# Two gated layers in split float32: every product as 64-row units in the two row tiles of TensorE

## What is computed

```python
x = causal_conv(x, softmax(weight, axis=-1))     # 4 x 4096 tokens of 192 features, 8 heads, 7 taps
h = x @ w_in1                                    # [16384, 192] @ [192, 2048]
x = (h * np.cos(h)) @ w_out1                     # [16384, 2048] @ [2048, 192]
h = x @ w_in2
out = (h * np.clip(h + 3.0, 0.0, 6.0) / 6.0) @ w_out2
```

## Time and profile before

| what | value |
|---|---|
| time, median of 3 runs | 2410.09 us (2410.08 to 2410.48) |
| the profiled execution's own time | 2408.54 us |
| its span, first to last instruction | 2406.8 us |
| mean granted clock of TensorE | 0.995 |
| matmuls | 10254 |
| weight loads | 10254 |
| DVE, ACT, POOL busy | 1776.7, 1495.7, 1313.7 us |
| moved by DMA | 32.8 MB, mean 14 GB/s |

### The profile page before, as it was taken

The page is one execution under the profiler, slowest core; times in us unless marked ns, Lnnn a source line. Parts: engine busy times, 40 slices in busy tenths (PEclk is TensorE's granted clock), DMA queues, the critical chain, the costliest instruction groups (busy, mean ns, idle before and its releaser), DMA issues.

```text
span 2406.8 us, 32826 instructions
## 1 busy us (share of the span) xinstructions
PE 2367.1 (98%) x10254; PEld 1929.2 (80%) x10254; DVE 1776.7 (74%) x2253; ACT 1495.7 (62%) x1748; POOL 1313.7 (55%) x543
## 2 busy tenths in 40 slices
PE   5999999999999999999999999999999999999998
PEld 3788888888888888888888888888888888888886
DVE  8777776777767777767777677777677776777753
ACT  4765566665666655666656666566666566665663
POOL 6755555555555555555555555555555555555554
PEclk8999999999999999999999999999999999999999
DMA  4100000000000000000000000000000000000001
GB/s 110 38 1 13 7 7 13 13 13 13 0 13 13 13 13 7 7 13 13 13 13 0 13 13 13 13 6 7 13 13 13 13 0 13 13 13 13 3 4 20
DMA packets 208226, 32.76 MB, mean 14 GB/s; under 512 B 203088, under 2 KB 207184, under 8 KB 208208
## 3 DMA queue, kind: packets, MB, share of 16 engines
q1 hardware_dynamic: 208208, 32.53, 7.7%
HBM read 19.92 MB, written 12.58 MB: 14 GB/s over the span
## 4 chain that ended last, share of the span: by engine, by line
PE 97%; DVE 1%; issue 1%; DMA 1%; SPq 0%; ACT 0%; POOL 0%; DVEq 0%; POOLq 0%; ACTq 0%
PE h_ps L347 10%; PE h_ps L346 10%; PE acc L366 10%; PE acc_tail L368 10%; PE h_ps L349 10%; PE acc L365 10%; PE acc_tail L369 10%; PE h_ps L348 10%; PE h_ps L350 10%; PE acc L367 10%; DMA gate<-in_moe_w_out 1%; DVE pre L520 0%; DVE gate L533 0%; DVE in_ftail L580 0%; DVE in_f L580 0%
## 5 line engine op out<-in xcount | busy, mean ns | idle before, releaser
L690 POOL TENSOR_TENSOR g_lo<-gate,g_hi 128x1024 fp32r<-128x1024 f32 x512 | 1270.2, 2481 | 1070.0 <-ACT g_hi L442 1069.7
L428 ACT ACTIVATE pre<-h_ps,three 128x1024 f32<-128x1024 f32 x256 | 286.7, 1120 | 547.0 <-PE h_ps L350 547.0
L442 ACT ACTIVATE g_hi<-gate 128x1024 fp32r<-128x1024 f32 x512 | 538.8, 1052 | 31.7 <-DVE gate L533 31.2
L520 DVE TENSOR_TENSOR pre<-pre,h_ps 128x1024 f32<-128x1024 int32 x256 | 311.9, 1218 | 257.3 <-ACT pre L426 257.3
L535 DVE SCALAR_TENSOR_TENSOR gate<-pre,h_ps 128x512 f32<-128x512 f32 x512 | 327.3, 678 | 214.5 <-ACT pre L428 213.5
L533 DVE TENSOR_TENSOR gate<-pre,h_ps 128x512 f32<-128x512 f32 x512 | 331.6, 685 | 129.4 <-ACT pre L436 126.0
L346 PE MATMUL h_ps<-in_hi,win_hi 128*128 128x512 f32 x1024 | 406.1, 397 | 18.7 <-DVE gate L533 9.9
L426 ACT ACTIVATE pre<-h_ps 128x1024 int32<-128x1024 f32 x256 | 262.4, 1025 | 232.5 <-PE h_ps L350 232.5
L347 PE MATMUL h_ps<-in_lo,win_hi 128*128 128x512 f32 x1024 | 406.1, 397 | 0.0
L349 PE MATMUL h_ps<-in_tail,wtail_hi 128*128 128x512 f32 x1024 | 403.4, 394 | 0.0
L366 PE MATMUL acc<-g_lo,wout 128*128 128x512 f32 x1024 | 402.6, 393 | 0.0
(11 more groups left out here) (69 smaller groups left out, 2225.8 us busy)
## 6 DMA issues: line engine op xcount, KB each, us to landing
x_in<-in_x SPq DMA_DIRECT2D x128, 64.0 KB, 2.2
out_dram<-o_blk SPq DMA_DIRECT2D x128, 64.0 KB, 1.8
blk_tail<-in_x SPq DMA_DIRECT2D x64, 64.0 KB, 2.2
out_dram<-blk_tail SPq DMA_DIRECT2D x64, 64.0 KB, 1.8
stage<-in_moe_w_out SPq DMA_DIRECT2D x6, 384.0 KB, 3.2
stage<-in_moe_w_in SPq DMA_DIRECT2D x3, 512.0 KB, 3.7
stage<-in_moe_w_in SPq DMA_DIRECT2D x6, 256.0 KB, 4.1
gate<-in_moe_w_out SPq DMA_DIRECT2D x2, 384.0 KB, 12.2
```

What stands on the lines that cost most here:

```text
L442: act.activation(g_hi[:, q % G_BUFS, :], gate[:, q % 2, :], ACT.Copy).then_inc(ghi_ready, 1)
L690: pool.tensor_tensor(g_lo[:, n, :], gate[:, q % 2, :], g_hi[:, n, :].bitcast(F32), ALU.subtract).then_inc(glo_ready, 1)
```

## The change

A matmul of 128 rows becomes two *units* of 64 rows: the lower ones use rows 64 to 127 (`LOW`), the upper ones rows 0 to 63 (`UP`), each with its own weight load. A slot has 19 *turns*; in each, a lower unit is issued and then an upper one, into different banks:

| turns | lower rows | upper rows |
|---|---|---|
| 0 to 2 | first product, half 0 (5 units, turns 0 to 4) | the last 3 tail units of the second product before |
| 3 to 8 | first product, half 1 (4 units, turns 5 to 8) | main second product, 6 units |
| 9 to 12 | tail of the second product, 4 units | first product, half 0, 4 units |
| 13 to 17 | main second product, 5 of its 6 units | first product, half 1, 5 units |
| 18 | the sixth | tail of the second product, its first unit |

The unit that would be low x low is left out: of 40 half-matmuls 38 stay. For that the low tail weights lie in one row half for even chunks and in the other for odd ones, and `in_twin` holds the tail's high part in rows 64 to 127. Four semaphores (`h_lower`, `tail_lower`, `main_upper`, `main_lower`) keep the two row tiles from working on one bank. `h_ready` now comes once per half, after turns 12 and 17; ACT, DVE and POOL work on 512 columns at a time throughout. `high_part` of slot q comes behind `cosine` of the same slot. The splits for layer 2 move to slots 1 to 5 of layer 1's phase (4 to 6 in the second phase of the kernel); the convolution goes three steps a slot from slot 1; the second products of the last three slots run by themselves at the end (`last_mixes`). `h_ps`, `acc` and `acc_tail` keep their sizes.

```diff
-        wtail_lo = [sb(f"wtail_lo{n}", [P, FF], F32R) for n in (1, 2)]
+        wtail_lo = [sb(f"wtail_lo{n}", [P, FF // 2], F32R) for n in (1, 2)]
...
+        in_twin = [sb(f"in_twin{n}", [P, TOK], F32R) for n in (1, 2)]
...
+                hi = wtail_hi[layer][:, cols]
+                lo = wtail_lo[layer][:, (i // 2) * HALF_FF // 2:(i // 2 + 1) * HALF_FF // 2]
+                return (src, hi), [(every_other(src, rows, odd), every_other(hi, rows, odd),
+                                    lo[rows, :].rearrange("p (c f) -> p c f", f=P))
+                                   for odd, rows in ((1, slice(0, DT)), (0, slice(DT, P)))]
...
-        SPLIT_SLOT = 4
+        SPLIT_SLOT = SLOTS - 2
         TURN_SLOT = SLOTS - 1
+        TURNS = 19
         STEPS_AHEAD = 4
         L1, L2 = 0, 1
+        SPLIT_EARLY = {"hi": 1, "twin": 2, "tail": 4, "low_main": 2, "low_tail": 5}
+        SPLIT_AFTER_DRAIN = {"hi": 4, "twin": 4, "tail": 5, "low_main": 5, "low_tail": 6}
...
-                          None if last else k + 1, 2, 4, 2 if first else None, L2)]
+                          None if last else k + 1, 1, 3, 2 if first else None, L2)]
...
+            def first_unit(rows, layer, source, q, half, n, start=False, stop=False):
+                c = slice((2 * q + half) * P, (2 * q + half + 1) * P)
+                if n < 3:
+                    w = (win_lo if n == 2 else win_hi)[layer][rows, c]
+                    x = (in_lo if n == 1 else in_hi)[source][rows, :]
+                elif n == 3:
+                    w, x = wtail_hi[layer][rows, c], in_tail[source][rows, :]
+                else:
+                    w = wtail_lo[layer][rows, q * P:(q + 1) * P]
+                    x = (in_twin if half == 0 else in_tail)[source][rows, :]
+                return pe.matmul(chunk_of(h_ps, q, half), w, x, start=start, stop=stop)
+            def main_unit(rows, layer, pair, q, n, start=False, stop=False):
+                half, part = divmod(n, 3)
+                cols = slice(D + DT, 2 * D) if part == 2 else slice(0, P)
+                g = chunk_of(g_lo if part == 1 else g_hi, q, half)
+                return pe.matmul(acc[pair][:, :], wout[layer][rows, 2 * q + half, cols], g[rows, :],
+                                 start=start, stop=stop)
+            def tail_unit(rows, layer, pair, q, n, start=False, stop=False):
+                half, part = divmod(n, 2)
+                g = chunk_of(g_lo if part == 1 else g_hi, q, half)
+                return pe.matmul(acc_tail[pair][:, :], wout[layer][rows, 2 * q + half, P:2 * P], g[rows, :],
+                                 start=start, stop=stop)
...
+            def lower(i, ph, q, slot, mix):
+                if i < 9 and ph is not None:
+                    half, n = (0, i) if i < 5 else (1, i - 5)
+                    if i == 0:
+                        source_waits(ph, q)
+                    if n == 0 and (ph.setup != 0 or q >= 2):
                         pe.wait_ge(g_ready, 2 * slot - 3 + half)
...
+                    last = first_unit(LOW, ph.layer, ph.source, q, half, n, start=n == 0)
+                    if i in (4, 8):
+                        last.then_inc(h_lower, 1)
+                if 9 <= i < 13 and mix is not None:
+                    layer, pair, mq = mix
+                    if i == 9 and not (isinstance(slot, int) and slot == LAG):
+                        pe.wait_ge(mix_done, slot - LAG)
+                    last = tail_unit(LOW, layer, pair, mq, i - 9, start=mq == 0 and i == 9)
+                    if i == 12:
+                        last.then_inc(tail_lower, 1)
+                if i >= 13 and mix is not None:
+                    layer, pair, mq = mix
+                    if i == 13:
+                        pe.wait_ge(main_upper, slot - LAG + 1)
+                    last = main_unit(LOW, layer, pair, mq, i - 13, stop=mq == SLOTS - 1 and i == 18)
+                    if i == 18:
+                        last.then_inc(main_lower, 1)
+            def upper(i, ph, q, slot, mix, left):
+                if i < 3 and left is not None:
+                    layer, pair, mq = left
+                    last = tail_unit(UP, layer, pair, mq, i + 1, stop=mq == SLOTS - 1 and i == 2)
+                    if i == 2:
+                        last.then_inc(mix_done, 1)
+                if 3 <= i < 9 and mix is not None:
+                    layer, pair, mq = mix
+                    if i == 3:
+                        if ph is not None:
+                            mix_waits(ph, q)
+                        if not (isinstance(slot, int) and slot == LAG):
+                            pe.wait_ge(main_lower, slot - LAG)
+                    if i in (3, 6):
+                        pe.wait_ge(ghi_ready, 2 * (slot - LAG) + i // 3)
+                        pe.wait_ge(glo_ready, 2 * (slot - LAG) + i // 3)
+                    last = main_unit(UP, layer, pair, mq, i - 3, start=mq == 0 and i == 3)
+                    if i == 8:
+                        last.then_inc(main_upper, 1)
+                if 9 <= i < 18 and ph is not None:
+                    half, n = (0, i - 9) if i < 13 else (1, i - 13)
+                    if n == 0:
+                        pe.wait_ge(h_lower, 2 * slot + half + 1)
+                    last = first_unit(UP, ph.layer, ph.source, q, half, n, stop=i in (12, 17))
+                    if i in (12, 17):
+                        last.then_inc(h_ready, 1)
+                if i == 18 and mix is not None:
+                    layer, pair, mq = mix
+                    pe.wait_ge(tail_lower, slot - LAG + 1)
+                    tail_unit(UP, layer, pair, mq, 0)
+            def mix_of(ph, q):
+                if q >= LAG:
+                    return ph.layer, pair_of(ph), q - LAG
+                return None if ph.setup == 0 else (ph.before, 1 - pair_of(ph), q - LAG + SLOTS)
...
+                    left = mix_of(ph, q - 1) if q > 0 else None
+                    if q == 0 and ph.setup != 0:
+                        left = ph.before, 1 - pair_of(ph), SLOTS - LAG - 1
+                    for i in range(TURNS):
+                        lower(i, ph, q, ph.base + q, mix_of(ph, q))
+                        upper(i, ph, q, ph.base + q, mix_of(ph, q), left)
+            def last_mixes():
+                layer, pair = L2, pair_of(last_phase())
+                for q in range(SLOTS - LAG, SLOTS):
+                    for i in range(TURNS):
+                        lower(i, None, q, END - SLOTS + q + LAG, (layer, pair, q))
+                        upper(i, None, q, END - SLOTS + q + LAG, (layer, pair, q), (layer, pair, q - 1))
+                for i in range(3):
+                    upper(i, None, None, None, None, (layer, pair, SLOTS - 1))
...
             def before_gate(layer, q, slot):
...
+                for half in range(2):
+                    act.wait_ge(h_ready, 2 * slot + half + 1)
+                    h, p = chunk_of(h_ps, q, half), chunk_of(pre, q, half)
+                    if layer == L1:
+                        i = act.activation(p.bitcast(I32), h, ACT.Copy, bias=0.25)
+                    else:
+                        i = act.activation(p, h, ACT.Relu, bias=three[:, 0:1])
+                    i.then_inc(pre_ready, 1)
             def cosine(q, slot1):
...
                 for half in range(2):
+                    act.wait_ge(frac_ready, 2 * slot1 + half + 1)
                     p = chunk_of(pre, q, half)
                     act.activation(p, p, ACT.Sin, bias=half_pi[:, 0:1], scale=-TWO_PI).then_inc(cos_ready, 1)
             def high_part(q, slot, reused):
...
                 if reused:
                     act.wait_ge(mix_done, slot - G_BUFS + 1)
...
+                for half in range(2):
+                    act.wait_ge(g_ready, 2 * slot + half + 1)
+                    act.activation(chunk_of(g_hi, q, half), chunk_of(gate, q, half),
+                                   ACT.Copy).then_inc(ghi_ready, 1)
...
+            def split_twin(layer, to):
+                act.activation(in_twin[to][DT:P, :], in_ftail[layer][:, :], ACT.Copy).then_inc(twin_ready[to], 1)
...
                     before_gate(ph.layer, q, slot)
...
                     if ph.layer == L1:
                         cosine(q, SLOTS * ph.tile + q)
...
+                    if ph.convolved is not None and q == SPLIT_SLOT:
                         act.wait_ge(conv_step, len(STEPS) * (ph.convolved + 1))
                         split_high(L1, L1)
                     if splits_last(ph, q):
                         act.wait_ge(acc_read, ph.number)
                         split_high(L2, L1)
+                    high_part(q, slot, ph.setup != 0 or q >= G_BUFS)
+                    if q == DRAIN_SLOT and ph.before is not None:
+                        copy_low(ph.before, 1 - pair_of(ph), ph.base, ph.number)
+                    if ph.layer == L1 and ph.setup != 0:
+                        if q == hands_over(ph)["hi"]:
```

(34 more changed lines are left out.)

191 lines of the change are left out of this document (67 added, 124 removed).

## The result

| | before | after |
|---|---|---|
| median of the runs, us | 2410.28 (2410.08 to 2410.66) | 2374.73 (2372.65 to 2375.52) |
| time of the profiled execution, us | 2408.5 | 2375.52 |
| span, us | 2406.8 | 2373.8 |

The ratio is 0.9851, with a 95% interval of 0.9834 to 0.9868: 35.5 us faster, inside the range, and a third of the 104 us that were forecast.

The account below looks back on a forecast made before the run. TensorE's matmuls were taken as the bound: 9785 turns x 0.2299 = 2249.6 us, plus 54.3 for start and end, 2303.9; with 1.6 from profiled execution to median 2305.5, say 2306 us. Range 2255 to 2485.

Parts of the forecast that it names:

- the turn: Part 1, TensorE: two units stream side by side, so a turn costs 0.2299 us, as a matmul does now; 9785 turns.
- the doubled handover: Rival, TensorE: each turn pays the weight handover twice, 0.245 us, 2453 us in all; chance 0.14 with milder and harsher forms.
- the exposed load: Rival, TensorE: the second tile waits for its weight load, a turn costs 0.34 us, 3383 us in all; chance 0.08.
- the serial units: Rival, TensorE: the units run one after another, most turns two units at 0.2299 us, some 4500 us; chance 0.06.
- issue: Rival, PE's queue: 76 instructions and about 12 waits a slot at 0.055 are 4.84 us, over 4.37: 2534 us; chance 0.05.
- if they go through one port: Part 1, weight loads: a turn's two loads take 2 x 0.11 = 0.22 us, under 0.23, so just hidden.
- the order within PE: Part 2: waits between row tiles look back at least three turns, 0.69 us against a matmul row of 0.40; taken 0.
- The cover of 0.3 us: Part 3, layer 1: peak lateness about 2.3 us against 2.6 us of room, so no stall of PE; taken 0.
- The rival that named a shortage of an elementwise engine: Layer 1's phases: ACT becomes the bound, PE stops 1 to 3.3 us in each of 31 tiles, 2337 to 2408; chance 0.10.
- Part 3: Half-width work on ACT, DVE and POOL: throughput and latency fit in both layers' phases, no stall of PE; taken 0.
- 4.0 of 5.75: Part 3, layer 2's phase: the split for the next phase, from slot 6, takes 4.0 of 5.75 us and ends in time.
- Sixty serial turns: Part 1, kernel's end: the last three second products run one after the other, 3 x 19 + 3 = 60 turns.

Follow-up runs that it names:

- experiment 5: The changed kernel, with POOL keeping its two 512-column instructions a slot but starting the first only when both halves of g_hi are there: 2313.13 us, ratio 0.9598.
- experiment 3: The changed kernel, with the next tile's transposition and halo copies moved from layer 2's phase to the last slot of layer 1's phase: 2375.26 us, ratio 0.9855.
- experiment 1: The changed kernel, with POOL's low part again one instruction of 1024 columns a slot instead of two halves: 2317.18 us, ratio 0.961.
- experiment 8: The kernel of experiment 1, with 128-row matmuls for the first products of the first three slots and the last three second products: 2313.63 us, ratio 0.9599.

## Why the prediction was right and wrong

**Right: the turn.** Taken 0.2299, measured 0.2312 (2150 us / 9300), 12.7 us in all. The break-even of 0.2406 was never near, and the rivals of the doubled handover (0.245), the exposed load (0.34), the serial units and of issue are out: PE stands for nothing in 2150 us of experiment 5. The prediction's "if they go through one port" did not come about: the two loads of a turn start 0.01 us apart, so there is no 0.22 to hide in 0.23. It changed no term. The Trainium skill (TensorE: Matmul & The Clock Gate, The mechanism) has, in its list of what overlaps, a load overlap a running matmul only where the row groups differ; the trace of after does not agree either, as in the pairs above the load of a row tile starts with that tile's own matmul, and the spacing stays 0.23.

**Right: the order within PE.** In the middle of experiment 5 no wait between the row tiles shows, as taken.

**Right: ACT in layer 1.** Behind its first turn, where PE waits for the input, no stop stands in layer 1's phases, with ACT at 30.89 of 36.07. The cover of 0.3 us held. The rival that named a shortage of an elementwise engine had the right kind of result (2337 to 2408) but the wrong engine, phase and line.

**Wrong: Part 3, on DVE.** The step is the sentence that DVE's "fuller phase is layer 2's, 30.58 of 36.80, to which nothing is added", with the 0 taken for it. No instruction is added, but 157 us of duration are, on two groups whose instructions did not change. Nor was the phase's new length set against it: 36.80 us became 35.1. Because the first half on POOL starts some 0.6 us sooner (one half of g_hi, 1.17 for two), it falls in front of DVE's convolution steps instead of behind them, and each step behind it is held by 1.04 us (experiment 5, which differs by this start alone, has 60 held steps for 210). DVE's share of layer 2's phase went to 33.13 of 36.40, and 61.9 us of stops came where 0 stood. Two readings would have shown it beforehand: in the earlier trace rows line 588 takes 2.61 us where the same shape takes 0.69 elsewhere, which the prediction saw and priced only as lateness in layer 1; and the means of line 580, 1063 and 795 ns against 0.73 us for a free step, which it does not use. They said that POOL and DVE hold each other, and then any move of POOL's start is a change to DVE.

The sentence on that phase's chain, "4.0 of 5.75", fell with it. Its durations held: the low part of the input took 0.68 and the one of the tail 0.69. What failed is that it began its count at slot 6 as if DVE came there on time, though the run of late work begins at slot 1 (experiment 3) and the last convolution step ends at 1016.36. Its result is wanted in PE at 1017.93, 1.6 us later, and the splits behind it take until 1019.21.

**Too high: the end.** Sixty serial turns were counted, 13.8 us; they took 10.7, as part of them ran side by side. With this and the longer turn, a kernel without stops was forecast at 2306 and came to 2313.13 in experiment 5.

So: the main effect was read to within 0.6%, the gain of the change to a third, since what was lost lay in an engine which was not the bound and had no instruction added in that phase. That the time still fell inside the stated range was no merit of the mechanism: the range took in losses that were argued for ACT and for a longer turn, not this one.

## What to carry to other kernels

Cutting an elementwise instruction in halves changes little in its cost (on POOL two of 1.29 us for one of 2.40) but moves its start, and with it which of two engines that hold each other comes first; look for one shape with two durations in the trace before taking a price, and let the engine with time to spare start second. Count the room of a nearly full engine from its last idle moment to the deadline and not as a share of a phase: work removed ahead of idle time buys nothing. When a stop in front of the bounding engine names an engine whose instructions are unchanged, look at what that engine's instructions overlap with.

## What the runs showed of the hardware that was not expected

- Two row tiles of 64 rows work side by side almost without loss: 0.2312 us for a pair against 0.2299 for one matmul of 128 rows, 1.99 units in the time of one, with loads that start 0.01 us apart.
- A stop of PE costs 0.10 us more than the stop: the turn behind it is 0.33 long.
- A DVE step with two inputs in SBUF is held for about 1.04 us by a POOL instruction of 512 columns that began 0.4 to 0.5 us before it, and by 2.2 (2.90 us in experiment 1, 60 times after 100 us) by one of 1024. The first steps (L683), which read one tensor and the taps, are held as well (1.5 for 0.47). When DVE is first, POOL is held instead (2.40 for 1.29).
- Where matmuls of 128 rows and of 64 follow each other (experiment 8), the first 64-row unit starts 0.32 us after the matmul ahead of it, the next one of 128 rows 0.43 after the unit, and the one behind that 0.34, in place of 0.23 each: 0.4 us for the way there and back.
